# At most two loads under way on SyncE, and the maximum of attention tile 5 ahead of the first lower half of g

## What is computed

```python
# attention: batch 2, 8 heads, 768 tokens, head width 64
for c in range(nc):
    scores = scale * np.matmul(q_c, k_full.transpose(0, 1, 3, 2))
    scores = scores - np.max(scores, axis=-1, keepdims=True)
    a = np.exp(scores)
    a = a / (np.sum(a, axis=-1, keepdims=True) + 1e-09)
    out[:, :, c_start:c_end] = np.matmul(a, v_full)
# dense layer: 1536 tokens, 512 wide, 2048 hidden
h = x @ w_in
g = h * (1.0 / (1.0 + np.exp(-1.702 * h)))
x = g @ w_out
# experts: 8, 512 wide, 1024 hidden, at most 384 tokens each
expert_idx = np.argmax(x @ w_gate, axis=1)
h = np.maximum(np.einsum('ecd,edf->ecf', disp, w1), 0.0)
y = np.einsum('ecf,efd->ecd', h, w2)
out[i] = gate_w[i] * y[expert_idx[i], pos[i]]
```

## Time and profile before

| | |
|---|---|
| runs before, us | 518.69 median of 3 (516.68 to 519.45) |
| profiled execution, us | 517.33, of which the span is 515.6 |
| granted TensorE clock, mean | 0.986 of 2.4 GHz |
| PE busy | 493.8 us, 96% of the span |
| DVE, ACT, POOL busy | 310.7, 220.0, 163.1 us |
| DMA | 76.93 MB, 149 GB/s on average |

### The profile page before, as it was taken

The page is one execution under the profiler, slowest core; times in us unless marked ns, Lnnn a source line. Parts: engine busy times, 40 slices in busy tenths (PEclk is TensorE's granted clock), DMA queues, the critical chain, the costliest instruction groups (busy, mean ns, idle before and its releaser), DMA issues.

```text
span 515.6 us, 9464 instructions
## 1 busy us (share of the span) xinstructions
PE 493.8 (96%) x3531; PEld 407.2 (79%) x3531; DVE 310.7 (60%) x677; ACT 220.0 (43%) x384; POOL 163.1 (32%) x190
## 2 busy tenths in 40 slices
PE   7878999999999999999999999999999999999993
PEld 4756888788888888788888778888988888888882
DVE  4345565544437777323777778864577878738750
ACT  3434545444232122113212355623457767847620
POOL 3300010100000000200000007335337999999942
PEclk9789999999999999999999999999999999999998
DMA  8996431269620000100322237313796987966100
GB/s 294 314 299 193 149 103 43 83 210 320 207 81 1 1 2 0 48 34 10 114 81 83 81 88 240 83 63 108 244 321 213 353 347 252 344 232 224 44 27 33
DMA packets 26719, 76.93 MB, mean 149 GB/s; under 512 B 5279, under 2 KB 5279, under 8 KB 26400
## 3 DMA queue, kind: packets, MB, share of 16 engines
q1 hardware_dynamic: 22656, 69.77, 41.5%
q0 software_dynamic: 4000, 6.32, 3.4%
HBM read 62.92 MB, written 19.96 MB: 161 GB/s over the span
## 4 chain that ended last, share of the span: by engine, by line
PE 82%; DVE 5%; issue 5%; ACT 3%; DMA 2%; DVEq 1%; SPq 0%; another core or an unknown queue 0%; POOL 0%; ACTq 0%; POOLq 0%
PE bank L1333 10%; PE bank L1334 9%; PE bank L1335 9%; PE bank L1377 8%; PE bank L1379 8%; PE bank L1378 8%; PE bank L1346 7%; PE bank L1610 3%; PE bank L1348 3%; PE bank L1324 2%; PE bank L1612 2%; PE bank L1613 2%; PE bank L1614 2%; PE bank L1289 2%; PE bank L1305 2%
## 5 line engine op out<-in xcount | busy, mean ns | idle before, releaser
L391 POOL TENSOR_TENSOR w_lo<-raw,w_hi 128x256 fp32r<-128x256 f32 x104 | 91.8, 917 | 12.7 <-ACT w_hi L375 12.6
L641 ACT ACTIVATE g<-bank 128x512 f32<-128x512 f32 x48 | 28.7, 599 | 135.6 <-PE bank L1335 135.6
L554 POOL DMA_INDIRECT dispatched_rows<-rows,slot_idx x12 | 12.9, 1071 | 219.3 <-DVE slot_idx L1049 216.6
L375 ACT ACTIVATE w_hi<-raw 128x1024 fp32r<-128x1024 f32 x80 | 82.0, 1049 | 0.2 <-issue 0.2
L391 DVE TENSOR_TENSOR w_lo<-raw,w_hi 128x1024 fp32r<-128x1024 f32 (+1 forms) x60 | 69.9, 1174 | 19.7 <-ACT w_hi L375 18.9
L1333 PE MATMUL bank<-x_hi,w_hi 128*128 128x512 f32 x192 | 77.8, 405 | 0.0
L1377 PE MATMUL bank<-w_hi,g_hi 128*128 128x512 f32 x192 | 77.2, 402 | 0.0
L1334 PE MATMUL bank<-x_lo,w_hi 128*128 128x512 f32 x192 | 76.4, 398 | 0.0
L1335 PE MATMUL bank<-x_hi,w_lo 128*128 128x512 f32 x192 | 76.1, 396 | 0.0
L1379 PE MATMUL bank<-w_hi,g_lo 128*128 128x512 f32 x192 | 75.8, 395 | 0.0
L1378 PE MATMUL bank<-w_lo,g_hi 128*128 128x512 f32 x192 | 75.8, 395 | 0.0
(11 more groups left out here) (154 smaller groups left out, 830.2 us busy)
## 6 DMA issues: line engine op xcount, KB each, us to landing
raw<-expert_units SPq DMA_DIRECT2D x64, 512.0 KB, 6.6
raw<-dense_units SPq DMA_DIRECT2D x16, 512.0 KB, 10.2
tile_in<-attention_tiles SPq DMA_DIRECT2D x12, 592.0 KB, 8.0
dispatched_rows<-empty SPq DMA_DIRECT2D x26, 257.0 KB, 7.9
slot_rows<-dispatched_rows SPq DMA_DIRECT2D x26, 257.0 KB
tile_in<-attention_tiles SPq DMA_DIRECT2D x12, 384.0 KB, 10.4
gate_rows<-gate_rows SPq DMA_DIRECT2D x2, 1024.0 KB, 5.1
out<-rows,e_token POOLq DMA_INDIRECT x16, 4.1
```

The costliest lines, as they stand in the source:

```text
L375: act.activation(w_hi[u % RING][:, :], raw[u % RING][:, :], ACT.Copy).then_inc(s_whi, 1)
L391: last = engine.tensor_tensor(w_lo[u % RING][:, part], raw[u % RING][:, part], w_hi[u % RING][:, part].bitcast(F32), ALU.subtract)
```

## The change

Two edits. On SyncE, three helpers wait until a load has landed, and the list of loads is written anew so that each load is issued only once the one before the last has landed; the loads are also put in the order in which they are used (queries and keys 3 ahead of values 0, values 1 ahead of unit 0, values 3 behind unit 0's landing). This holds for the start and for the loop over tiles 4 to 11; the loads behind it are as before. On VectorE, `maximum(5, 0)` and `less_max(5, 0)` move in step 0 from behind `g_low(0)` and `split_lo` of unit 2 to the place between `gated(0)` and `g_low(0)`. PE's, ScalarE's and GpSimd's programs are unchanged.

```diff
-            for t in range(LEAD):
-                load_queries_keys(t)
+            def landed_queries_keys(t):
+                sp.wait_ge(s_qk[t % NSLOT], 16 * (t // NSLOT + 1))
+
+            def landed_values(t):
+                sp.wait_ge(s_v[t % NSLOT], 16 * (t // NSLOT + 1))
+
+            def landed_unit(u):
+                sp.wait_ge(s_raw[u], 16)
+
+            load_queries_keys(0)
+            load_queries_keys(1)
+            landed_queries_keys(0)
+            load_queries_keys(2)
+            landed_queries_keys(1)
+            load_queries_keys(3)
+            landed_queries_keys(2)
             load_values(0)
-            load_queries_keys(LEAD)
+            landed_queries_keys(3)
+            load_values(1)
+            landed_values(0)
             load_unit(0)
-            for t in range(1, FIRST):
-                load_values(t)
+            landed_values(1)
+            load_values(2)
+            landed_unit(0)
+            load_values(3)
+            landed_values(2)
             load_queries_keys(FIRST)
+            landed_values(3)
             load_unit(1)
+            landed_queries_keys(FIRST)
             load_queries_keys(FIRST + 1)
+            landed_unit(1)
             unit = 2
             for t in range(FIRST, NT):
                 load_unit(unit)
-                unit += 1
+                if t + 1 < NT:
+                    landed_queries_keys(t + 1)
                 load_values(t)
+                landed_unit(unit)
                 if t + 2 < NT:
                     load_queries_keys(t + 2)
+                landed_values(t)
+                unit += 1
...
                 gated(i)
+                if i == 0:
+                    maximum(FIRST + 1, 0)
+                    less_max(FIRST + 1, 0)
                 g_low(i)
...
-                if FIRST < t + 2 < NT:
+                if FIRST + 1 < t + 2 < NT:
                     maximum(t + 2, 0)
                     less_max(t + 2, 0)
```

## The result

The changed kernel takes 511.78 us (median of 8 runs, 510.51 to 513.3). The kernel before took 517.01 us in the runs beside it (median of 8, 515.32 to 519.45). The ratio is 0.989, 95% interval 0.9866 to 0.9914: 5.2 us faster by the medians. Forecast were 508.3 us and, against its own profiled execution, a gain of 9.5 us. The direction was right and the measured time lies in the range, but only a little over half of the gain came.

What follows compares the result with a forecast made beforehand. PE was taken as bound by its late entry into the regular pace: stops 5.05, clock 4.0 and VectorE 1.96 make 11.0 us, less 1.5 for loads 9.5; 517.33 becomes 507.8, plus 0.5 gives 508.3 us, range 505.7 to 513.8.

Steps and rivals of the forecast that it cites:

- (a), the stops: PE's two instruction-fetch stops, 2.38 and 2.67 us, go but for 0 to 1 us; fetches wait 2 to 3 us, not 6.
- The rival that the fetch doesn't care: Load queue depth doesn't hold PE's fetch; stops and clock stay, only VectorE's 1.96 us is gained: 515.4 us, chance 0.09.
- the prediction's reading: Of the skill's round-robin rule: queued loads hold a fetch for one packet only; limiting loads gives nothing beyond 1.96 us.
- (c), VectorE: In step 0, the earlier maximum and `less` of tile 5 remove PE's wait at 40.64 us: 1.96 us gained.
- (b), the clock: PE's two stretches at 1.2 GHz each follow a stop; with the stops gone, full clock returns 4.0 us.
- What is late next: Loads, at 2.1 us each, bring tile 5's queries and keys at 27 us, wanted at 25.6: 1.5 us lost.
- The bounds: One load's share with two in flight, as half its latency: 1.9 us (values alone), 2.95, or 3.4 (behind two others).
- The estimate by the page of the Trainium skill: 2.0 us plus bytes over 436 GB/s: 3.4 us per 592 KB load, share 1.7, full 11.0 us gain; not used.
- Slack in the steps: In the regular steps each load has over a step of slack; unit 7, issued some 3 us later, costs nothing.

Runs made afterwards that it cites:

- one load: The changed kernel with one load under way at a time instead of two, one look: 550.49 us.
- The loads alone: The changed kernel with VectorE's step as before, so only the new load list and its waits: ratio 0.9935, 514.71 against 517.83 us.
- VectorE alone: The changed kernel with the old load list and no waits, so only VectorE's moved step: ratio 0.9935, 514.36 against 517.83 us.
- the second one: A second profiled execution of the unaltered changed kernel, from its repeat beside other kernels on one chip: median 513.32 us, ratio 0.9909 to the kernel before.

## Why the prediction was right or wrong

*(a), the stops: right.* Both went, and the fetch delay with two loads, 2.4 to 3.3 us, is in the 2 to 3 us (at most 0.3 over) that I had worked out from the bytes in flight. The rival that the fetch doesn't care is refuted: the same order of loads has the stops without the limit and not with it. The working from bytes is not confirmed with that. Other traces with two loads have 0.9 to 3.5 us, and one load, which has fewer bytes in flight, has 5.7 once. That the forecast size fits this one trace is in part luck.

This also bears on the rule of the Trainium skill that a DMA engine changes queue rows after each packet ("DMA: Bandwidth & Descriptors", Queues, rings and completion order). The prediction took it to mean that a fetch is hardly held at all. The page's packet is several descriptors, typically 9 to 17, and no run here shows how many of the trace's packets make one of them. So the delays of 4.1 to 6.2 us speak against the prediction's reading, but don't settle the rule.

*(c), VectorE: right, a little low.* The loads alone keep a wait of 2.09 us, the changed kernel has none. By time VectorE alone gave 3.5 us; the forecast 1.96 is just inside the interval, whose lower end is 1.9.

*(b), the clock: half right.* Of the 4.0 us the matmuls gave back 2.56. With the loads alone the clock stayed at 2.4 GHz up to the transposes, and the same matmuls took 26.15 us; against that the low clock cost 4.5 us before and 2.0 after. The first dense group runs at full clock in every profile with the move or the limit, but for the one with one load. But I tied the low stretches to the stops alone; a wait for a load of 1.8 us was followed by one just as well (18.3 to 25.1 us). And whether it comes differs from one execution of the same kernel to the next: the second one waited 1.7 us at the same place and stayed at full clock.

*What is late next: right in kind, wrong in size.* This is the step that failed. I took 2.1 us for a load from rows in which loads overlapped; it is 2.45. That is the smaller part: ten loads by 0.35 are 3.5 us at tile 5. The larger fault is that I charged the loads once, at `scores(5)`, 1.5 us. That very group doesn't wait at all (30.80, right behind the first dense group). The loads were late for five groups before it: `scores(1)` 0.33, `scores(2)` 1.54, `scores(3)` 1.13, `values(1)` 1.80, `values(2)` 0.28, and for ScalarE's split of unit 0 by 1.65. The first dense matmul came at 27.85 and not between 22.7 and 25. Where 0.7 us of such waits stood before there are now 5.1, so the limit cost 4.4 us and not 1.5.

The missing 4.1 us (9.5 less 5.4, by the spans) add up. Idle time of PE up to the transposes should have shrunk by 5.05+1.96-1.5 = 5.51 and shrank by 3.34: 2.2 us, the 2.9 too little for loads less some short waits that went. The clock is 1.4 us, 4.0 less 2.56. The last 0.5 us are behind the transposes.

*The bounds: too kind.* The lowest row (3.8/2 = 1.9) was a load with nothing in front. Two loads in flight don't halve that: each has 0.95 us without a packet at its start, and at its end a stretch with few engines at work. The estimate by the page of the Trainium skill, 1.7 us for a load, is further off still; its fit is for DMAs issued by GpSimd, and these are issued by SyncE. Here too the trace decides.

*Slack in the steps: wrong.* Unit 3, issued at 34.61, took 4.05 us, ScalarE waited 0.30 for it, and through its split PE waited 0.5 us for `less` at 44. In the second execution it was 1.22 and 1.35 us. So a better clock or an earlier start could bring this kernel nothing more as long as unit 3 landed at 38.6. The prediction gave each load in the steps more than a step of slack, and named unit 7 alone.

## What to carry to other kernels

A limit on the loads under way is a dial, not a switch: count what it takes from the late instruction fetches and what it gives to late loads at each of its settings, and expect the best between the ends (here three or four, which are not told apart, where two came first). Where a change makes a resource thinner, charge it at every consumer on the path in order of time, and not at the last one. A split of the same number of matmuls into idle and busy time tells gaps and clock apart at once. And when an earlier start brings nothing, look for the load further on whose landing has not moved.

## What the runs showed of the hardware

An instruction fetch can come 6 us after PE has entered the block: 4.1 to 6.2 us with no limit on the queued loads, 0.9 to 3.5 with two under way, and 5.7 once with one. PE then goes on about 2.6 us after the fetch's packet has begun (27.1 to 29.65, 11.2 to 13.77 in the kernel before). With two loads in flight the 16 DMA engines are busy for 0.69 of the first 34.7 us, at 209 GB/s, against 0.98 and 301 without a limit. The Trainium skill states that the next block of 16 KB is fetched while the current one runs, and that crossing a boundary is mostly hidden ("Runtime: NRT & Kernel Launch", Instruction fetch mechanics). The records agree on blocks of 256 instructions: the places where PE stops lie 256 or 512 records apart, and each packet of queue 8 is of 16 KB. Hidden it is in the regular steps, but not in the first 30 us without a limit, where PE stopped for 2.38 and 2.67 us.
